# Four VectorE operations change places in the first phase of an attention and expert kernel: low parts of h, a maximum, late joins and masks, and one early join

## The reference

```
for t in range(S):                      # S = 768, 4 batches, 8 heads, D = 48
    S_re, S_im = ar*S_re - ai*S_im + k_t v_t^T, ar*S_im + ai*S_re
    y[t] = q_t @ S_re
h = max(y @ w1, y @ w2, y @ w3)         # 3072 tokens, 384 -> 768
x2 = h @ w_out                          # 768 -> 384
# then a top-1 choice among 8 experts, 384 -> 1024 -> 384 each, scaled by the gate
```

## Time and profile before

| | us |
|---|---|
| median of 3 runs | 923.27 (922.94 to 923.33) |
| the profiled execution, own time | 924.32 |
| its span | 922.5 |
| TensorE, VectorE, ScalarE, GpSimd busy | 809.4, 658.0, 442.1, 519.9 |

### The profile page before, as it was taken

One profiled execution on the slowest core, in us unless ns is written; L12 is line 12 of the kernel. 1 busy time (PEld: TensorE's weight loads), 2 busy tenths in 40 slices (PEclk: granted clock), 3 DMA queues, 4 the chain that ended last, 5 costly groups with the idle time before them and its releaser, 6 DMA issues.

```text
span 922.5 us, 18638 instructions
## 1 busy us (share of the span) xinstructions
PE 809.4 (88%) x6641; PEld 745.6 (81%) x6642; DVE 658.0 (71%) x1066; ACT 442.1 (48%) x817; POOL 519.9 (56%) x886
## 2 busy tenths in 40 slices
PE   0567888898988988999899999958999999999995
PEld 0445787887877877888798999947999999998894
DVE  5988879998997988898978776367532263647831
ACT  5685846664644565656544444232221142436611
POOL 1199999799999999898978000002422332324222
PEclk9769989999999999999999999976999999999998
DMA  9401142452424242414131120443611123326311
GB/s 303 124 20 33 48 127 74 115 149 74 115 74 109 75 109 74 110 57 102 59 80 49 43 64 26 156 148 126 234 43 34 59 95 131 122 94 246 112 35 43
DMA packets 41874, 89.72 MB, mean 97 GB/s; under 512 B 6264, under 2 KB 23680, under 8 KB 40480
## 3 DMA queue, kind: packets, MB, share of 16 engines
q1 hardware_dynamic: 37632, 76.04, 27.2%
q0 software_dynamic: 4160, 12.60, 4.1%
HBM read 69.74 MB, written 17.69 MB: 95 GB/s over the span
## 4 chain that ended last, share of the span: by engine, by line
PE 50%; DVE 19%; POOL 17%; issue 8%; ACT 3%; DMA 2%; ACTq 0%; DVEq 0%; SPq 0%; POOLq 0%
POOL c_im L2095 5%; PE yu L1723 4%; POOL c_re L2094 4%; PE yu L1727 4%; PE yu L1724 4%; POOL ring L2098 4%; PE mm L1723 4%; PE mm L1727 3%; POOL ring L2097 3%; PE mm L1724 3%; PE yu L1768 2%; PE tr L1995 2%; PE mm L1995 2%; PE mm L1997 2%; PE tr L1996 2%
## 5 line engine op out<-in xcount | busy, mean ns | idle before, releaser
L1723 PE MATMUL mm<-up_hi,x_hi 128*128 128x384 f32 x432 | 158.6, 367 | 11.4 <-DVE h_sb L1181 10.8
L1724 PE MATMUL mm<-up_lo,x_hi 128*128 128x384 f32 x432 | 148.5, 344 | 0.0
L2094 POOL TENSOR_TENSOR c_re<-ring 112x128 f32<-112x128 f32 x165 | 103.6, 628 | 62.5 <-DVE ring L1134 36.6
L2095 POOL TENSOR_TENSOR c_im<-ring 112x128 f32<-112x128 f32 x165 | 123.3, 747 | 0.0
L2174 POOL DMA_INDIRECT out_rows<-g_o,rows_out x30 | 36.2, 1206 | 146.3 <-DVE g_o L1575 134.3
L1727 PE MATMUL mm<-up_hi,x_lo 128*128 128x384 f32 x432 | 101.3, 343 | 2.2 <-DVE x_lo L1169 2.2
L1723 PEld LDWEIGHTS mm<-up_hi,x_hi 128*128 128x128 f32 x432 | 83.3, 193 | 19.2 <-DVE h_sb L1181 13.5
L2098 POOL TENSOR_TENSOR ring<-c_re,c_im 112x64 f32<-112x64 f32 x165 | 96.4, 584 | 0.0
L1181 DVE TENSOR_TENSOR h_sb<-mm,h_sb 128x384 f32<-128x384 f32 x96 | 52.8, 550 | 58.3 <-PE mm L1727 58.3
L2150 POOL DMA_INDIRECT g_in<-x_scratch,rows_in x34 | 37.8, 1112 | 95.4 <-DVE rows_in L1538 69.9
L2097 POOL TENSOR_TENSOR ring<-c_re,c_im 112x64 f32<-112x64 f32 x165 | 83.8, 508 | 12.9
(11 more groups left out here) (263 smaller groups left out, 2266.4 us busy)
## 6 DMA issues: line engine op xcount, KB each, us to landing
raw<-in_moe_w SPq DMA_DIRECT2D x16, 1536.0 KB, 9.6
a_dn<-in_a_laid SPq DMA_DIRECT2D x18, 384.0 KB, 7.0
an_scratch<-a_dn SPq DMA_DIRECT2D x18, 384.0 KB, 2.3
ring<-an_scratch SPq DMA_DIRECT2D x18, 384.0 KB, 5.8
q_in<-in_q_laid SPq DMA_DIRECT2D x24, 224.0 KB, 2.7
k_in<-in_k_laid SPq DMA_DIRECT2D x24, 224.0 KB, 3.0
v_in<-in_v_laid SPq DMA_DIRECT2D x24, 192.0 KB, 3.1
x_scratch<-x_sb SPq DMA_DIRECT2D x24, 192.0 KB, 1.9
```

The lines of the kernel that those rows point to most:

```text
L1723: nc.tensor.matmul(out, hi[:, x, :], w_hi(x), start=(x == 0), stop=False)
L1724: nc.tensor.matmul(out, hi[:, x, :], w_lo(x), start=False, stop=False)
L2094: nc.gpsimd.tensor_tensor(c_re[:, 0:count, :, :], cur, bc(prev[:, :, 0, :], 2, 2), ALU.mult).then_inc(chain_prod, 1)
L2095: nc.gpsimd.tensor_tensor(c_im[:, 0:count, :, :], cur, bc(prev[:, :, 1, :], 2, 2), ALU.mult).then_inc(chain_prod, 1)
```

## The change

Only VectorE's list and one function that ScalarE reads too are touched. `mask(n)` moves behind `moe_h_lo(n-2, 1)` in the chunks other than 1, 3 and 5. The first early join moves ahead of `moe_max(n-1, 0, 1)`; a second early join (chunks 6 and 8) moves behind `moe_max(n-1, 0, 2)`. `maxima_first` becomes true for chunks 9 to 20 too, so `moe_max(n-1, 1, 1)` stands ahead of the late join and `norm_inverse` there, and ScalarE's `norm_rest` of those chunks (9 to 16, which have one) moves behind x_hi of the next. `moe_h_lo(n-1, 0)` follows that maximum ahead of the late join in all chunks that have one. Nothing is added or removed.

```diff
         def maxima_first(n):
-            return n in joins_late and n < 9
+            return n in joins_late
...
                 for m in norms[:1]:
                     norm_m2(m, norm_of(m))
-                if now and not late_z:
-                    mask(n)
                 if prev2:
                     moe_h_lo(n - 2, 1)
                 if n in (3, 5):
                     for g, number in early:
                         join(g, number)
-                if now and late_z:
+                if now:
                     mask(n)
...
+                for g, number in early[:1] if not late_z else ():
+                    join(g, number)
                 if prev:
                     moe_max(n - 1, 0, 1)
-                for g, number in early if not late_z else ():
-                    join(g, number)
...
                 if prev:
                     moe_max(n - 1, 0, 2)
+                for g, number in early[1:] if not late_z else ():
+                    join(g, number)
...
                 if maxima_first(n):
                     moe_max(n - 1, 1, 1)
+                    moe_h_lo(n - 1, 0)
                 for g, number in late:
                     join(g, number)
                 for m in norms:
                     norm_inverse(m, norm_of(m))
                 if prev and not maxima_first(n):
                     moe_max(n - 1, 1, 1)
-                if prev:
                     moe_h_lo(n - 1, 0)
```

## The result

The changed kernel takes **913.32 us** (median of 4 runs, 912.38 to 914.45) against 923.27: a ratio of 0.9893, with an interval of 0.9876 to 0.9911. That is 9.9 us faster (8 to 11.5), where 8.3 had been summed and 915.0 forecast; 913.32 is just inside the lower edge of the forecast's own range, 913.3 to 916.8. The profiled execution had 913.05 of its own, with a span of 911.3.

A forecast was written before the change was run, and what follows sets the result against it. Bounds: GpSimd's chains to 296.50 us, a VectorE-TensorE loop to 474.30, then TensorE. Terms 2.5 + 0.93 + 1.4 + 0.4 + 2.4 + 0.7 = 8.3 us gave 915.0 us; own range 913.3 to 916.8, full range 912.0 to 920.6.

The forecast's parts named there:

- What bounds the kernel.: To 296.50 us GpSimd's chains, hiding VectorE's gains up to chunk 9; then the VectorE-TensorE loop; from 474.30 TensorE.
- Chunk 2 and chain 4.: Chunk 2: shorter TensorE stop, full clock, chain 4 starting 4.1 us earlier, chain 6 ending 2.5 us earlier; bounds 0 and 4.1.
- The old stop had a second price: Chunk 2: clock 0.50 behind the 2.88 us stop, 1.00 behind chunk 8's 2.40; a 1.68 us stop should keep it up.
- The slowing of the chains.: Chains 4 to 6: each us of VectorE's work costs GpSimd about 0.4 us, taking 1.6 from the 4.1 us.
- Other edits before chunk 9: Chunks 6 and 8, one early join moved: frees TensorE up to 2.5 us each, hidden by the wait for chain 6.
- Chunk 9, 0.93.: Chunk 9: third maximum and h_lo fill the wait for the chain, so the fourth maximum comes 0.93 us earlier.
- Even chunks and chunk 12.: The join fills VectorE's wait for group 1: 1.4 us for chunks 10, 14, 16; 2.4 us for chunk 12.
- Odd chunks.: Chunks 11 to 17: path from fourth maximum through h_hi shortens 0.1 us each, 0.4 in all; bounds -0.4 and 1.6.
- Chunks 18 on.: TensorE bounds; its stops of 0.51 us at 489.79 and 0.17 in the next chunk go: 0.7 us.
- The rival on ScalarE: norm_rest and z_t copies make each h_hi 0.4 us later: about 3 us gain left, 920.3 us; chance 0.12.
- GpSimd as the pace: Chains 4 to 11 lengthen as VectorE hardly idles; slower from 43.0 us a chain, 931 at 44; chance 0.07.
- The other signs.: Profile: chain 4 without DMA wait, VectorE waiting for h_hi up to 0.5 us in chunks 10 to 17, L1754 stops replacing L1768's.

The follow-up runs named there:

- the run with the join moved: Changed kernel with the first join of pair 6 moved from chunk 9 to chunk 10, ahead of the first maximum: 914.67 us, ratio 0.9909.
- the swap: Mask placed behind h_lo in chunk 2; added alone to the kernel before: 920.78 us, ratio 0.9985.
- early joins alone: Kernel before with only the first early join ahead of the first maximum and the second behind the second maximum: 917.69 us, ratio 0.9952.
- swap left out: Changed kernel with mask ahead of h_lo again in chunk 2 alone: 914.14 us, ratio 0.9908.
- second join back: Changed kernel with the second early join of chunks 6 and 8 right behind the first maximum again: 914.05 us, ratio 0.9896.
- norm_inverse first: Changed kernel with norm_inverse ahead of the late join in chunk 9 alone: 913.08 us, ratio 0.9894.
- ScalarE's old order: Changed kernel with norm_rest ahead of the next x_hi again in chunks 9 to 17, VectorE's list kept: 918.65 us, ratio 0.9953.
- h_hi first: Changed kernel with norm_inverse ahead of chunk 9's late join and, from chunk 9, h_hi of half 1 ahead of two z_t copies: 912.93 us, ratio 0.9898.
- The run with the stop of 4.27 us: Changed kernel with mask and rotation of chunk 2 ahead of h_lo: 916.19 us, ratio 0.9942.
- the two with only its later parts changed: Kernel before plus only third maximum and h_lo ahead of late joins, norm_rest behind x_hi (920.10 us); kernel before plus only the early-join moves (917.69 us).

## Why the forecast held, step by step

**What bounds the kernel.** Right for before. That what VectorE gains up to chunk 9 is waited away there was right too, and wider than told: the run with the join moved shows that it holds up to chunk 13 in the changed kernel.

**Chunk 2 and chain 4.** The profile bore it out nearly number by number: a stop of 1.63 us (1.68 foreseen), clock 1.00, group 1 at 119.45 without a wait, the second maximum at 123.57 (123.9), chain 4 at 167.30 (168.3), VectorE waiting 3.08 us in chunk 4. As a term for the median it is this step that failed, and in one sentence: "The old stop had a second price". It took the low clock of one execution for a fixed price of the old stop. In the five profiles with a stop of 2.6 us or more at this place the clock fell behind stops of 2.88, 2.90 and 4.27 us and stayed behind 2.62 and 2.85; in all nine with the swap (stops of 1.40 to 1.69) it stayed. So here the swap goes with a clock that stays up, where without it the clock falls in some executions. The 2.97 us measured up to the join of chunk 9 don't bear out the term either: without the swap, but with a clock that stayed up, that join comes at 293.02 (early joins alone) and 293.11 us (swap left out), earlier than the 293.58 of the changed kernel. They are the distance to an execution whose clock fell. In the runs the swap is worth 1.4 us whichever way it is taken, added alone or left out alone (9.9 less 8.5), against the term's 2.5; the intervals reach from nothing to 3 and over. The median came out right all the same, as the rest, without the swap, is worth 8.5 us where the other terms had 5.8. That the sum is off by only 1.6 us is in part luck, as the two misses have opposite signs.

The other sentence of that step, "A stop of 1.68 lies below both, so I take it that the clock stays up", came true nine times, but its reason doesn't hold. In chunk 3, whose lists are as before, TensorE stops for 1.78 to 1.80 us at one place. Timeline and stretch, first of the changed kernel, then of the one with the second join back:

```profile
149.16 0.45 PE L1723 MATMUL mm<-up_hi,x_hi 128*128 128x384 f32 x1 [1.80 <-DVE h_sb L1181]
...
149.10:153.10 4.00, 3.94 (x25) 3.66 (x27) 3.90 (x7) 1.62 (x4) 3.92 (x4) 1.00 0.16 44
```

```profile
150.12 0.45 PE L1723 MATMUL mm<-up_hi,x_hi 128*128 128x384 f32 x1 [1.78 <-DVE h_sb L1181]
...
150.10:154.10 4.00, 3.98 (x15) 3.89 (x16) 3.90 (x6) 1.57 (x3) 3.92 (x4) 0.59 0.18 35
```

The kernel before (1.78 us) and that with norm_inverse first (1.79 us) fell there too, to 0.60 and 0.57. So a stop far shorter than 2.40 us can have a fall behind it, and the same code falls in one execution and not in the next.

The Trainium skill, page "TensorE: Matmul & The Clock Gate", section "Part 1: The HAM clock gate (the warmup mystery)", has the clock fall back through idleness. The traces agree in kind; stops of 2.85 and 2.88 us, and of 1.80 and 1.78, on either side of the fall show that the length of one stop didn't decide it here.

**The slowing of the chains.** 0.4 us of GpSimd's time for each us of VectorE's work was the estimate. From chain 4's start to chain 7's it was 124.27 us and is 126.41, beside VectorE's 111.20 and 115.53 us: 2.1 for 4.3, or 0.5. The 1.6 of the sum measured 2.1, and the 4.1 ahead of it 5.1. One pair of executions can't fix this rate. From chain 4's start to chain 7's the runs with ScalarE's old order, with the second join back, with norm_inverse first and with h_hi first took 124.70, 125.49, 127.11 and 127.23 us, beside 113.94, 115.42, 117.58 and 117.10 us of VectorE's work. Against the 124.27 and 110.92 of before that is 0.1, 0.3, 0.4 and 0.5. What the estimate was not carried into is chains 7 and 8, which lost 4.1 us.

Single steps show how it comes about. Timelines of GpSimd and of VectorE in the changed kernel, end of chain 8:

```profile
376.39 1.33 POOL L2094 TENSOR_TENSOR c_re<-ring 112x128 f32<-112x128 f32 x1
377.67 0.46 POOL L2095 TENSOR_TENSOR c_im<-ring 112x128 f32<-112x128 f32 x1
```

```profile
376.16 1.23 DVE L1250 TENSOR_TENSOR k_t<-z_t,k_in 112x1024 f32<-112x1024 f32 x1
377.32 0.55 DVE L1181 TENSOR_TENSOR h_sb<-mm,h_sb 128x384 f32<-128x384 f32 x1
377.79 0.54 DVE L1186 TENSOR_TENSOR h_lo<-tr,h_hi 128x384 fp32r<-128x384 f32 x1
```

Beside L1250, which reads two tensors in SBUF, a product that can take 0.46 us takes 1.33 and ends 0.3 us behind it; beside a maximum, which reads one of its inputs from the bank `mm`, and the h_lo behind it, which reads one from the bank `tr`, the next product takes 0.46. The Trainium skill, page "SBUF — State Buffer", section "Who interferes with whom", has such a lock for VectorE instructions with two SBUF inputs beside a GpSimd read. These rows agree with it. The 4 us that the prediction worked out by it as a bound were not reached; that only part of VectorE's instructions are of that kind would explain it, but no run separates them.

**Other edits before chunk 9 are hidden.** Right, by the run with the second join back.

**Chunk 9, 0.93.** Exact. norm_inverse stayed behind the join; put ahead of it, chain 8 started 0.9 us earlier in the profile of that run.

**Even chunks and chunk 12.** Right in cause and nearly in size (1.94 for 1.4, 2.26 for 2.4); the waits for group 1 are gone, as foreseen.

**Odd chunks.** 1.16 for 0.4, and unevenly: chunk 11 gave 0.99, as the upper bound allowed for, and chunk 13 took 0.28 back through the wait for chain 8. That h_hi ends 3.3 us behind the fourth maximum was right: in chunk 15 it is 407.85 - 404.57 = 3.28. The working listed "x_hi, 0.41, is now done before" as a small help on this path. Its real weight was the 5.6 us (4.2 by the profiles) of the run with ScalarE's old order.

**Chunks 18 on.** 1.25 for 0.7; the small remainder was not followed up.

**The rivals.** The rival on ScalarE had the right place. Its condition, h_hi 0.4 us later, did not come in the changed kernel, but the run with ScalarE's old order has it and measured 918.65. The prediction's 920.3 for it was added up wrongly: by its own terms 2.5 + 0.93 - 0.8 + 2 + 0.7, some 5.3 us are left and not 3, which gives 918.0. GpSimd as the pace came true from 296.5 to about 420 us without making the kernel slower: chains 4 to 10 take (463.14 - 167.30) / 7 = 42.3 us each, under the 43.0 from which it would have decided, and near the 42.6 worked out. The wait for GpSimd in chunk 13, 0.52 us, is one of the signs that was to prove the forecast wrong; it cost the last part of the gain, not the gain.

**The other signs.** The clock and the stop in chunk 2, the waits in chunks 4 and 9, the missing waits for group 1 in the even chunks and the change of place from L1768 to L1754 came as named. Chain 4 still waits 0.53 us for its DMA. VectorE waits for h_hi in chunk 17 alone (0.50 us), not in chunks 10 to 16; it is TensorE that waits for h_hi, by 0.60 us in each of chunks 11 to 17.

## What to carry to other kernels

A time read from one profiled execution may hold a price that not every execution pays: where a term rests on a fallen clock, look for a second trace of the same code before it is credited to an edit. When two engines' lists are tightened, follow the third engine that works beside them: its pace is not a constant, and here it slowed as the others stood less (two chains took 85.1 us after 81.0). And where a function steers two engines, follow every instruction that stands in line behind the one that waits longer; here about half the gain hung on x_hi not standing behind norm_rest.

## What was not expected of the hardware

With the same code up to chunk 2, the kernel before and the two with only its later parts changed had 0.50, 0.50 and 1.00 there, behind stops of 2.88, 2.90 and 2.62 us. The two that fell, and no other kernel without the swap, also had a clock of 0.86 or 0.85 between 90 and 100 us. Two kernels with the swap (second join back, h_hi first) had 0.86 there as well and kept 1.00 in chunk 2, behind stops of 1.69 and 1.67 us. The run with the stop of 4.27 us fell with 1.00 between 90 and 100. So the dip ahead of it may belong to the cause, but neither it nor the stop decides alone. What does isn't settled.

Chunk 2 is not the only such place. The changed kernel's own profile has a clock of 0.50 from 169.9 to 173.9 us, behind a stop of 2.65 us in chunk 4, where VectorE now waits for chain 3; that of before has 1.00 there, and falls of its own in chunks 3, 5 and 6 (0.60, 0.65 and 0.59 over 4 us). A profile as a whole thus holds several such falls, and comparing two of them compares these too. The kernel with the swap alone ran from 918.53 to 925.30 us and the one before, beside it, from 920.10 to 925.27, so the fall in chunk 2 is not all that makes executions differ.

In the changed kernel a stop of 5.07 us behind the join of chunk 9 has a clock of 0.50 behind it for 4 us; before, the stop there was 4.01 us with 0.57 behind it. The path lies on GpSimd there; what this fall costs was not taken apart from the stop itself.
